# A scan of token levels made in place for two chunks at once, its inner levels as 64x64 matmul tiles

## What is computed

```python
for t in range(S):
    kt, vt, rt, wt = (k[:, :, t], v[:, :, t], r[:, :, t], w[:, :, t])
    cur = np.einsum('bhd,bhe->bhde', u[None] * kt, vt)
    y[:, :, t] = np.einsum('bhd,bhde->bhe', rt, state + cur)
    state = wt[:, :, :, None] * state + np.einsum('bhd,bhe->bhde', kt, vt)
...
ch = np.maximum(xn @ w_ch1, 0.0) @ w_ch2                          # first block, xn normalised
h = np.maximum(x @ w_in, 0.0)                                     # second block
v_s = np.einsum('ts,bsd->btd', w_spatial, v_n) + b_spatial[None, :, None]
out = (u * v_s) @ w_out
```

## Time and profile before

| | us |
|---|---|
| median of three runs | 480.67 (480.61 to 480.84) |
| the profiled execution: its time | 481.9 |
| the profiled execution: its span, first to last instruction | 480.1 |
| of it the attention, until the first matmul of the second stage | 182.3 |
| of it the second stage | 297.8 |
| TensorE busy over the span | 436.2 (91%) |
| VectorE, ScalarE, GpSimd busy | 244.6, 234.0, 139.2 |

### The profile page before, as it was taken

One profiled execution on the slowest core, in us unless ns is written; L12 is line 12 of the kernel. 1 busy time (PEld: TensorE's weight loads), 2 busy tenths in 40 slices (PEclk: granted clock), 3 DMA queues, 4 the chain that ended last, 5 costly groups with the idle time before them and its releaser, 6 DMA issues.

```text
span 480.1 us, 7972 instructions
## 1 busy us (share of the span) xinstructions
PE 436.2 (91%) x2724; PEld 415.4 (87%) x2724; DVE 244.6 (51%) x564; ACT 234.0 (49%) x570; POOL 139.2 (29%) x198
## 2 busy tenths in 40 slices
PE   3688777877888889999999999999999999999997
PEld 3588777866777879999999999999999998899997
DVE  6887889886777863125432431334241674403120
ACT  4888898888898883322222322332221752211111
POOL 6475765656656672500000000100010530000000
PEclk9979999998899989999999999999999999999999
DMA  7424343243332121200000000000500110010102
GB/s 205 153 72 123 96 122 86 72 125 101 115 111 72 34 59 35 66 1 1 1 0 1 2 0 1 0 1 0 194 5 1 33 34 2 0 51 0 51 2 96
DMA packets 26539, 25.49 MB, mean 53 GB/s; under 512 B 1666, under 2 KB 21890, under 8 KB 26500
## 3 DMA queue, kind: packets, MB, share of 16 engines
q1 hardware_dynamic: 26500, 24.99, 18.0%
HBM read 22.62 MB, written 2.36 MB: 52 GB/s over the span
## 4 chain that ended last, share of the span: by engine, by line
PE 77%; issue 9%; DVE 7%; ACT 5%; DMA 1%; SPq 0%; DVEq 0%; ACTq 0%
PE bank L1150 20%; PE bank L1152 19%; PE bank L1151 19%; PE bank L1055 11%; ACT rz L586 2%; DVE score L802 2%; PE bank L1128 2%; DVE rin L781 1%; ACT score L642 1%; PE bank L1099 1%; PE bank L1112 1%; PE bank L1098 1%; PE bank L1235 1%; DVE wtot L762 1%; DMA kin<-in_kT 1%
## 5 line engine op out<-in xcount | busy, mean ns | idle before, releaser
L1055 PE MATMUL bank<-rz,k 128*128 128x128 f32 x576 | 86.9, 298 | 32.2 <-issue 24.6
L1055 PEld LDWEIGHTS bank<-rz,k 128*128 128x128 f32 x576 | 76.3, 206 | 40.2 <-issue 33.0
L586 ACT COPY rz<-rin 64x256 f32<-64x256 f32 x144 | 58.4, 405 | 19.6 <-DVE rin L781 18.2
L524 POOL TENSOR_TENSOR vrstd<-vmv,half 128x1 f32<-128x1 f32 x12 | 7.7, 642 | 156.6 <-DVE vmv L1001 156.6
L802 DVE COPY_PREDICATED score<-msk,bank 128x512 f32<-128x512 int32 x48 | 50.1, 1044 | 0.6
L781 DVE TENSOR_TENSOR rin<-rin,wtot 128x256 f32<-128x256 f32 x60 | 27.3, 455 | 33.5 <-ACT rz L586 32.7
L507 POOL TENSOR_TENSOR k<-k,wtot 128x256 f32<-128x256 f32 x60 | 43.0, 717 | 3.8 <-ACT k L611 1.3
L690 ACT ACTIVATE h10h<-bank 128x384 fp32r<-128x384 f32 x24 | 11.8, 490 | 50.1 <-PE bank L1152 50.1
L918 DVE SCALAR_TENSOR_TENSOR h11l<-bank,h11h 128x384 fp32r<-128x384 f32 x24 | 13.4, 558 | 37.7 <-ACT h11h L690 37.7
L918 DVE SCALAR_TENSOR_TENSOR h10l<-bank,h10h 128x384 fp32r<-128x384 f32 x24 | 13.4, 558 | 35.7 <-ACT h10h L690 35.7
L611 ACT COPY k<-k 128x256 f32<-128x256 f32 x72 | 29.5, 410 | 2.4 <-POOL k L505 0.6
(11 more groups left out here) (159 smaller groups left out, 1177.7 us busy)
## 6 DMA issues: line engine op xcount, KB each, us to landing
stage<-in_w SPq DMA_DIRECT2D x12, 384.0 KB, 3.2
vin<-in_v SPq DMA_DIRECT2D x12, 288.0 KB, 2.9
rin<-in_rT SPq DMA_DIRECT2D x12, 256.0 KB, 4.6
win<-in_wT SPq DMA_DIRECT2D x12, 256.0 KB, 3.7
kin<-in_kT SPq DMA_DIRECT2D x12, 256.0 KB, 4.3
out<-ob SPq DMA_DIRECT2D x12, 192.0 KB, 1.9
stage<-in_w_in SPq DMA_DIRECT2D x4, 384.0 KB, 3.2
x<-in_w_sp SPq DMA_DIRECT2D x4, 384.0 KB, 4.7
```

Of the source, the lines that this page charges most:

```text
L586: last = sc.copy(dst, src[lo:hi, :, :, :])
L1055: mm = te.matmul(b_level[n % 3][:, a * P:(a + 1) * P], kk[:, a, :], rz[l][:, a, :, :].rearrange("p e t -> p (e t)"), start=True, stop=True)
```

## The change

**In place.** `rin` and `kin` are now multiplied where they lie: `r_right` and `k_left` write back into them, and the copies `pad`, `k_right` and `k_pairs` and the tiles `rz`, `k_2` to `k_128` are gone. So both now wait for the level's matmuls to have read r and k, and the next level waits for both.

**Two chunks in step.** The lists go by steps s = 0 to 12, each of four slots j: the low levels (1, 2, 4, 8) of chunk s stand in the slots beside the high ones (16, 32, 64) of chunk s-1. Low and high levels have two PSUM banks each (`low`, `high`), which are written again at every level, after their scores were taken.

**Tiles of 64x64.** Levels 1 to 32 are made inside blocks of 64 tokens (`near_level`): for each pair of heads, each block and each head one matmul of 64 partitions, 64 weight columns and 32 streamed columns, 16 to a level. The term of a token with itself is 16 more with 64 streamed columns (`own_term`), on `uk`, which ScalarE makes as k times u. Level 64 is 8 matmuls with 64 streamed columns (`far_level`). `gain` is 8 matmuls of 64 weight columns. `attend` takes 4 + 8 matmuls of 128 weight columns. The weights are 128x128 nowhere but in `attend` and the transposes.

**Masks.** VectorE takes the term of a token with itself (128x512) and all six levels (128x256 each) into `near`, one of two tiles of [128, 8, 64]; ScalarE copies `near` and level 64 into the one `score` tile. The state is kept narrow and spread into `wide` by ScalarE. The decays of chunks 2 on are made for two chunks in one instruction, which waits for both chunks' w.

The diff, cut to its core:

```diff
+Q = 64
+N_LOW = 4
+N_HIGH = NL - N_LOW
+N_MASKED = 6
+N_MIDDLE = N_MASKED - N_LOW
...
-        rz = [place(f"rz{l}", [P, NPR, 2, P // 2]) for l in range(NL)]
-        score = [place(f"score{q}", [P, H, P]) for q in range(2)]
...
+        kin = [place(f"kin{q}", [P, NPR, P]) for q in range(4)]
+        win = [place(f"win{q}", [P, 2 * NPR, P]) for q in range(2)]
+        vin = [place(f"vin{q}", [P, H, HD]) for q in range(3)]
+        wtot = [place(f"wtot{q}", [P, 2 * NPR, P]) for q in range(2)]
+        wend = [place(f"wend{q}", [P, 2 * NPR, 1]) for q in range(2)]
+        uk = place("uk", [P, NPR, P])
+        near = [place(f"near{q}", [P, H, Q]) for q in range(2)]
+        score = place("score", [P, H, P])
+        kt = place("kt", [P, NPR, P])
+        state = place("state", [P, NPR, HD])
...
+        wide = place("wide", [P, NPR, 2 * HD])
...
+        low_bank = ctx.enter_context(nc.psum_tensor("low_bank", [P, 2, BANK], F32))
+        high_bank = ctx.enter_context(nc.psum_tensor("high_bank", [P, 2, BANK], F32))
+        low = low_bank[:, :, :].rearrange("p e (a t) -> p (e a) t", t=P)
+        high = high_bank[:, :, :].rearrange("p e (a t) -> p (e a) t", t=P)
...
             def load_w(i):
                 b, c = i // CH, i % CH
-                if i >= 2:
-                    sp.wait_ge(k_left_ready, NL * (i - 2) + 1)
-                    sp.wait_ge(r_ready, NL * (i - 2) + 1)
-                    sp.wait_ge(decays_ready, NL * (i - 2) + 1)
-                sp.dma_start(win[i % 2][:, :, :], wT[b, :, :, c * P:(c + 1) * P]).then_inc(w_in_sbuf[i % 2], 16)
+                if i >= 4:
+                    k_ready(sp, i - 4, 0)
+                    r_ready(sp, i - 4, 0)
+                    sp.wait_ge(decays_ready, decay_count(i - 4, 0))
+                sp.dma_start(win[i // 2 % 2][:, NPR * (i % 2):NPR * (i % 2 + 1), :],
...
-                s_, d_ = halves(src[:, :, :], c)[0], halves(kc[2 * c][:, :, :], c)[0]
-                wr = run_ends(wt(q, c), 1)
+                    pool.wait_ge(decays_ready, decay_count(i, n - 1))
+                    k_ready(pool, i, n - 1)
+                level_done(pool, i, n)
+                k = halves(kin[i % 4][:, :, :], c)[0]
+                wr = run_ends(wt(i, c), 1)
...
-            def pad(i, l):
...
-            def k_right(i, n):
...
+            def place_near(i):
+
+                act.wait_ge(middle_placed, N_MIDDLE * (i + 1))
+                act.wait_ge(low_placed, N_LOW * (i + 1))
+                act.wait_ge(own_placed, i + 1)
+                if i:
+                    act.wait_ge(y_done, i)
+                else:
+                    act.wait_ge(score_zeroed, 1)
+                for s0 in range(0, P, Q):
+                    last = sc.copy(score[s0:s0 + Q, :, s0:s0 + Q], near[i % 2][s0:s0 + Q, :, :])
+                last.then_inc(near_placed, 1)
...
+            def widen(i):
+
+                act.wait_ge(state_ready, carried(i))
+                if i == 0:
+                    act.wait_ge(wide_zeroed, 1)
+                act.wait_ge(y_done, i + 1)
+                for e, (lo, hi) in enumerate(HALF):
+                    last = sc.copy(wide[lo:hi, :, e * HD:(e + 1) * HD], state[lo:hi, :, :])
+                last.then_inc(wide_ready, 1)
...
             def decays(i, n):
 
-                q, c = i % 2, LEVELS[n]
+                i0, count = decay_unit(i)
+                c = LEVELS[n]
                 if n == 0:
+                    for m in range(i0, i0 + count):
+                        w_loaded(dve, m)
+                    if i0 >= 4:
+                        k_ready(dve, i0 - 3, NL - 1)
+                        r_ready(dve, i0 - 3, NL - 1)
+                else:
...
+            def r_right(i, n):
+
+                c = LEVELS[n]
+                if n:
+                    dve.wait_ge(decays_ready, decay_count(i, n - 1))
+                    r_ready(dve, i, n - 1)
+                else:
...
+                level_done(dve, i, n)
...
+            def own_select(i):
+
...
+                if i >= 2:
+                    dve.wait_ge(near_placed, i - 1)
+                dve.wait_ge(own_done, i + 1)
+                dve.wait_ge(low_done, N_LOW * i + 1)
+                mk = msk[:, N_MASKED * Q // 2:]
+                ve.copy_predicated(near[i % 2][:, :, :], mk[:, None, :].to_broadcast([P, H, Q]),
+                                   low[:, :, Q:2 * Q]).then_inc(own_placed, 1)
+
+            def select(i, n):
+
+                c = LEVELS[n]
+                if n == 0:
+                    dve.wait_ge(own_placed, i + 1)
+                elif n <= N_LOW:
+                    dve.wait_ge(low_placed, N_LOW * i + n)
+                else:
+                    dve.wait_ge(middle_placed, N_MIDDLE * i + n - N_LOW)
+                level_done(dve, i, n)
+                src = (low if n < N_LOW else high)[:, :, 0:Q // 2]
+                mk = msk[:, n * Q // 2:(n + 1) * Q // 2]
...
+                at_slot = N_LOW * s + j
+                for i in range(4, NT, 2):
+                    n = at_slot - (N_LOW * (i - 2) + 3)
+                    if 0 <= n < NL:
+                        return [(i, n)]
+                return []
...
+            for s in range(NT + 1):
+                for j in range(N_LOW):
+                    if s < NT:
+                        r_right(s, j)
+                    if s >= 1 and j < N_HIGH:
+                        r_right(s - 1, N_LOW + j)
+                    if j == 0 and s < NT:
+                        own_select(s)
+                    if s < NT:
+                        select(s, j)
+                    if j < N_MIDDLE and s >= 1:
+                        select(s - 1, N_LOW + j)
+                    for i, n in decay_plan(s, j):
+                        decays(i, n)
+                    if j == 0:
+                        if 3 <= s < 3 + TG:
+                            norm(s - 3)
+                        if s >= 2 and carries(s - 2) and not first(s - 2):
+                            decay_state(s - 2)
+                    if j == 1 and s >= 2 and carries(s - 2):
+                        next_state(s - 2)
...
+            def own_term(i):
...
+                    for s0 in range(0, P, Q):
+                        for e, (lo, hi) in enumerate(HALF):
+                            mm = te.matmul(low[s0:s0 + Q, NPR * e + a, Q:2 * Q], uk[lo:hi, a, s0:s0 + Q],
+                                           rin[i % 4][lo:hi, a, s0:s0 + Q], start=True, stop=True)
+                mm.then_inc(own_done, 1)
+
+            def near_level(i, n):
+
+                c = LEVELS[n]
+                if n:
+                    r_ready(te, i, n - 1)
+                    k_ready(te, i, n - 1)
+                if 1 <= n < N_LOW:
+                    te.wait_ge(low_placed, N_LOW * i + n)
+                elif n > N_LOW:
+                    te.wait_ge(middle_placed, N_MIDDLE * i + n - N_LOW)
+                elif n == N_LOW and i:
+                    te.wait_ge(blocks_placed, i)
+                dst = low if n < N_LOW else high
+                for a in range(NPR):
+                    for s0 in range(0, P, Q):
+                        for e, (lo, hi) in enumerate(HALF):
+                            r = rin[i % 4][lo:hi, a, s0:s0 + Q].rearrange("p (m two c) -> p m two c", two=2, c=c)
+                            mm = te.matmul(dst[s0:s0 + Q, NPR * e + a, 0:Q // 2], kin[i % 4][lo:hi, a, s0:s0 + Q],
+                                           r[:, :, 1, :], start=True, stop=True)
+                mm.then_inc(low_done if n < N_LOW else high_done, 1)
...
+                te.wait_ge(middle_placed, N_MIDDLE * (i + 1))
+                for a in range(NPR):
+                    for t0 in range(c, P, 2 * c):
+                        for s0 in range(t0 - c, t0, Q):
+                            for e, (lo, hi) in enumerate(HALF):
+                                mm = te.matmul(high[s0:s0 + Q, NPR * e + a, 0:c], kin[i % 4][lo:hi, a, s0:s0 + Q],
+                                               rin[i % 4][lo:hi, a, t0:t0 + c], start=True, stop=True)
...
+                for a in range(NPR):
+                    for e, (lo, hi) in enumerate(HALF):
+                        mm = te.matmul(b_turn[lo:hi, a * HD:(a + 1) * HD], kt[:, a, lo:hi], vin[i % 3][:, 2 * a + e, :],
+                                       start=True, stop=True)
+                mm.then_inc(gain_done, 1)
...
+            for s in range(NT + 1):
+                for j in range(N_LOW):
+                    if s < NT:
+                        if j == 0:
+                            own_term(s)
+                        near_level(s, j)
+                    if s >= 1 and j < N_MIDDLE:
+                        near_level(s - 1, N_LOW + j)
+                    elif s >= 1 and j < N_HIGH:
+                        far_level(s - 1, N_LOW + j)
+                    if j == 0 and s >= 2 and carries(s - 2):
+                        gain(s - 2)
+                    if j == 2 and 3 <= s < 3 + TG:
```

(6 more changed lines are left out.)

637 lines of the change are left out of this document (236 added, 401 removed).

## The result

The changed kernel takes **542.1 us** (median of 4 runs, 539.5 to 542.5), the kernel before 480.8 (480.6 to 482.2) beside it: the ratio (time over that of the kernel before) is 1.126, interval 1.121 to 1.130. It is slower by 61 us. The forecast of 561.4 lay 19 us above it, inside its range and with the right sign. The sum behind it is another matter: three of its terms were off by 14 to 68 us each, and that they cancelled in part was luck.

A forecast was written before the change was run, and what follows sets the result against it. Attention was taken as bound by a round through several engines, the second stage by TensorE's matmuls. Steps of 21.3 us (16.6 work, 4.8 waits) gave attention 263.0 instead of 182.3, hence 561.4 us; range 477 to 650, chance 0.80.

The forecast's parts named there:

- The forecast's ordinary step: One attention step with both chunks: TensorE work 16.6 us plus exposed waits 4.8, giving 21.3 us, eleven times.
- 240 tile pairs: TensorE's 64x64 load-and-matmul pairs in a step, at 0.056 us each: 13.4 us.
- mask waits of slots 0 to 2, with `gain` and matmul tails: TensorE's exposed rounds in a step while levels wait for masks of the shared low bank: 4.8 us.
- second stage: The two feed-forward blocks, bound by TensorE's own matmuls, which the change leaves alone: stays at 298 us.
- The price of a pair: Spacing of 64x64 tile loads on TensorE: 0.056 us, half of 0.111, going with the weight columns; chance 0.50.
- wrong if tile loads start 0.03 apart or less: One of the forecast's own signs of failure, on TensorE's tile loads, which it expected to start 0.056 us apart.
- The rival that takes both savings, 0.014: TensorE tiles: load and overlap both shrink, 0.014 us a pair, step 11.3, attention 153.6, total 452 us; chance 0.12.
- The clock: TensorE's clock falling to its lower level in longer waits: counted at nothing, TensorE being busier than now.
- The queue for w: VectorE's decays wait for the later chunk's w: covered at 0.056 a pair, 1.5 us late four times at 0.028.
- The masks: Each low level waits for the previous slot's mask: rounds of 2.1, 1.4 and 1.2 us in slots 0 to 2.
- The halves of the masks: VectorE's masks at half as many elements: 0.65 us and about 0.43 us.
- the rival with tiles side by side: Four TensorE tiles at once, 0.028 us a pair: step 14.6, attention 188.4, total 487 us, range 477 to 497; chance 0.17.

The follow-up runs named there:

- other runs with TensorE busy for 90 and 99.6 of 100 us: Changed kernel with second low bank pair, earlier w, `turned_lo` ahead of decays: 513.6 us; kernel of 464.7 us with dead products on one array corner: 519.4 us.
- The kernel of 464.7 us: Changed kernel plus second low bank pair, earlier w, `turned_lo` ahead of decays, dead products, turned x in y's bank one slot earlier: 464.7 us, ratio 0.964.
- the run that took 485.5 us: Changed kernel plus second low bank pair, w loaded a step earlier, `turned_lo` ahead of the decays, and dead products (the three together): 485.5 us, ratio 1.008.
- Dead work: Unread matmuls on a constant tile, 16 at start and 3 after slots 0 to 2; the same kernel took 464.7 us with them, 503.0 us without.

## Why the forecast was right in sign and wrong in its terms

The forecast's ordinary step was 21.3 us; the step shown above took 17.7, the others without a wait for `turned_lo` 17.2 to 19.0, and all eleven 19.6 on average. Its pairs are 125.28 to 128.00 (own term and two levels) and then 1.96, 2.0 and 1.04 us up to the next wait or `attend`, less three matmul tails, put at 0.17 each near the forecast's 0.16 (an estimate); it is one of the two steps without `turn_k`, whose 0.71 is from other steps.

| term of a step | forecast | measured |
|---|---|---|
| 240 tile pairs | 13.4 | 7.2 |
| `attend` | 2.7 | 5.3 |
| `turn_k` | 0.47 | 0.71 |
| mask waits of slots 0 to 2, with `gain` and matmul tails | 4.8 | 5.2 |
| all three waits for `turned_lo`, in the whole kernel | 0 | 13.6 |
| second stage | 297.8 | 300.0 |

**The price of a pair** was the step that failed first. The forecast took 0.056 since "nothing in these rows shows two loads running at once", and put the bound at 0.028 with four tiles side by side. (Its own rows have loads that last 0.192 and start 0.111 apart, so their records do overlap.) Measured: 0.024 at the lower clock, 0.0137 at the full one, with 0.066 for the same corner. The error is (13.4 - 7.2) x 11 = 68 us too much. By its own sign, "wrong if tile loads start 0.03 apart or less", the forecast's working was refuted, though its total held. The rival that takes both savings, 0.014, had the right price at full clock. The rule that the forecast quoted from the Trainium skill, "TensorEngine Tiling (Array Packing)", Key Properties (tiles load and multiply in parallel), is what this case shows. The Trainium skill's figure of some 60 cycles a matmul (the same page, section Instruction Overhead) is not the price of a tile pair in such a stream: 0.0137 us are 33 cycles of 2.4 GHz, for a load and a matmul together. For one corner by itself it is not contradicted, since each corner's turn comes after four pairs, 0.055 us. Nor did that figure of the Trainium skill speak for the prices above 0.056, as the forecast had it: 60 cycles of 2.4 GHz are 0.025 us, an estimate from the page's figure.

**The clock** was the term counted at nothing, for a reason that proved wrong: "TensorE is busier at 0.056 than now". It stood at 0.50, and stayed there in other runs with TensorE busy for 90 and 99.6 of 100 us. That doubled `attend` (2.6 us a step), made the turning of k longer, kept tile pairs at 0.024 instead of 0.0137 (240 x 0.0105 = 2.5 us a step), and slowed the first 5 us of the second stage. `attend` and `turn_k` alone are 2.6 x 11 + 0.24 x 10 = 31 us too little in the forecast.

**The queue for w** was followed to the right place and not to the end. The forecast had w late by 1.5 us at a small price of a pair and named r and the masks as what stands behind it. VectorE stood 6.3 us for it in step 4. The masks behind it cost some 3 us in the whole kernel; the dearer thing behind it was `turned_lo`, an instruction of another part of the kernel, with TensorE's turning of k behind that: 13.6 us, of which the earlier w took 6.4 away. I had listed who waits on VectorE's queue, but not who else uses the bank.

**The masks** were right, in place and about in size: 1.21, 1.39, 1.05 us of waiting behind 1.1 of `gain`, against 2.1 - 0.9, 1.4 and 1.2. The halves of the masks too: 0.72 and about 0.43 to 0.49. GpSimd's product, expected at 0.717, took 0.877, and still TensorE waited for it for under 3 us in all. VectorE's load per step, under 10 us, was right.

So 68 us too much, and 31 + 14 + 2 us too little, with some 4 more in the masks: 561.4 came within 19 us of 542.1 because errors that have nothing to do with each other cancelled. That is luck, and the sign is in part luck too. The exposed masks were a right reason for it. The price of the pairs was not: with the measured 7.2 us for them the forecast's own step would be 7.2 + 2.7 + 0.47 + 4.8 = 15.2 us (an estimate) against a period of 15.0 before, which is hardly a change. What made the kernel slower beyond that are terms that the sum had at nothing. The range held because its lower end was set by the rival with tiles side by side; of the 55 us between that rival's 487 and the measured time, 47 are these 31, 14 and 2. The kernel of 464.7 us, which has neither fault and a second pair of low banks besides, lies near the 452 of the rival on the faster side.

What made the change slower by 61 us is shown by taking it away: 29.7 us for the clock, 20.2 for the one pair of low banks and 14.7 for the shared bank, each alone, and 56.6 for the three together.

## What to carry to other kernels

Small tiles on different corners of the array are as cheap as their number promises only if the order of the loops visits the corners in turn, and they can cost the clock for everything else on TensorE: before packing matmuls into tiles, ask what full-size work is left in each stretch, and price full-size matmuls there at the lower clock too. Read the clock from the spacing of a known matmul, not only from its column. Where a buffer or a bank is shared, follow not only who stands behind a waiting instruction in its queue, but every user of what that instruction frees.

## What the runs showed of the hardware

- A 64x64 load with its matmul of 32 columns: 0.0137 us apart on four corners in turn at full clock, 0.024 at the lower one, and 0.066 on one corner at the lower one. With 64 weight columns on all rows (`gain`) it is 0.047 at the lower one. The step from one clock to the other is 1.8 and not 2; full-size loads went from 0.111 to 0.213, 1.9.
- TensorE at 90 and 99.6% busy with mostly 64x64 tiles stood at 1.2 GHz for 100 us. With nine added matmuls of 512 columns a step on the whole array it stood at 2.4 GHz; with nine of the same length on a quarter of the array it did not. In the run that took 485.5 us it was at the lower level behind pauses of 1.9, 2.8 and 2.3 us before the turning of k, even with them.
- Dead work paid: 38 us gained net, in a kernel where it took some 9 x 0.2 us a step. A burst of it at the start alone gave nothing (542.7 us).
- A masked copy of 128x256 took VectorE 0.72 us at the levels of 1 and 2 tokens and 0.43 at that of 4; one of 128x512 without gaps took 0.72.
- Not tried: dead work in the kernel before, whose attention has a clock of 0.95 and so has much less to win, and a second pair of banks for the high levels, for which no bank is left.
